# The ninth block of each probability tile: stored, and transposed together with those of other tiles

## The reference

```python
q_pool = q.reshape(B, H, S // 2, 2, D).mean(axis=3)
scores = scale * np.matmul(q_pool, k.transpose(0, 1, 3, 2))
scores = scores - np.max(scores, axis=-1, keepdims=True)
attn = np.exp(scores)
attn = attn / (np.sum(attn, axis=-1, keepdims=True) + 1e-09)
return np.matmul(attn, v)
```

## Time and profile before

| | us |
|---|---|
| Median of three runs | 989.16 |
| The profiled execution: device time | 988.49 |
| The profiled execution: span, first to last instruction | 986.7 |
| One pair, step 10 to step 10 (305.07 to 341.91) | 36.84 |
| TensorE busy in the span | 891.1 (90%) |
| VectorE busy | 597.8 (61%) |
| ScalarE busy | 497.0 (50%) |
| GpSimd busy | 294.5 (30%) |

### The profile page before, as it was taken

How to read it: one execution, slowest core, us unless ns; L and a number is a source line. 1 busy time by engine, 2 the same in 40 slices (tenths; PEclk the granted TensorE clock), 3 DMA queues, 4 the chain that set the end, 5 groups by cost and what they waited for, 6 DMA issues and landing times. The chain is left out here.

```text
span 986.7 us, 16399 instructions
## 1 busy us (share of the span) xinstructions
PE 891.1 (90%) x5707; PEld 644.4 (65%) x5707; DVE 597.8 (61%) x1175; ACT 497.0 (50%) x711; POOL 294.5 (30%) x207
## 2 busy tenths in 40 slices
PE   3999999999999999999999998876672899999998
PEld 2776776776776776776776765633231788888887
DVE  4676677677677677677677664420017866676770
ACT  1655555555555555555555553210016766666660
POOL 4353333333433333433433200000001343333441
PEclk9999999999999999999999999979885899999999
DMA  3312202202202202202202000949933100000000
GB/s 120 131 31 74 72 2 72 72 0 72 72 0 72 72 0 72 72 0 72 72 0 72 25 1 2 350 171 395 400 134 128 54 22 21 21 21 21 21 21 33
DMA packets 48865, 75.50 MB, mean 77 GB/s; under 512 B 5056, under 2 KB 23488, under 8 KB 48320
## 3 DMA queue, kind: packets, MB, share of 16 engines
q1 hardware_dynamic: 48832, 75.06, 22.3%
HBM read 70.32 MB, written 4.72 MB: 76 GB/s over the span
## 5 line engine op out<-in xcount | busy, mean ns | idle before, releaser
L496 DVE TENSOR_REDUCE part_neg<-ps 128x1 f32<-128x512 f32 (+1 forms) x432 | 220.8, 548 | 6.9 <-PE ps L304 6.6
L320 PE MATMUL ps<-ident,prob 128*128 128x128 f32 x1296 | 204.7, 285 | 19.1 <-DVE probT L415 9.2
L320 PEld LDWEIGHTS ps<-ident,prob 128*128 128x128 f32 x1296 | 143.2, 140 | 105.9 <-DVE probT L415 38.6
L415 DVE COPY probT<-ps 128x512 f32<-128x512 f32 (+1 forms) x256 | 125.1, 489 | 143.2 <-PE ps L320 116.8
L542 ACT ACTIVATE prob<-ps,neg_max 128x1152 f32<-128x1152 f32 x144 | 175.5, 1219 | 58.7 <-DVE neg_max L500 58.3
L304 PE MATMUL ps<-kT,qT_hi 128*128 128x512 f32 (+1 forms) x480 | 175.9, 383 | 5.3 <-DVE qT_lo L205 5.2
L553 ACT ACTIVATE probT<-ps 128x512 f32<-128x512 f32 x144 | 86.0, 597 | 171.6 <-PE ps L320 169.8
L337 PE MATMUL ps<-probT,v_nat 128*64 128x256 f32 (+1 forms) x1152 | 167.5, 417 | 0.5 <-DVE probT L415 0.5
L304 PE MATMUL ps<-kT,qT_lo 128*128 128x512 f32 (+1 forms) x480 | 159.3, 355 | 0.0
L1089 POOL TENSOR_TENSOR g_lo<-g,g_hi 128x1024 fp32r<-128x1024 f32 x36 | 86.5, 2404 | 134.7 <-ACT g_hi L1059 134.7
L1032 PE MATMUL ps<-w_hi,g_hi 128*128 128x512 f32 x288 | 113.9, 396 | 3.0 <-POOL g_lo L1089 3.0
(11 more groups left out here) (142 smaller groups left out, 1000.0 us busy)
## 6 DMA issues: line engine op xcount, KB each, us to landing
ring<-in_moe_w SPq DMA_DIRECT2D x10, 2048.0 KB, 20.1
k_nat<-in_k SPq DMA_DIRECT2D x16, 576.0 KB, 4.0
v_nat<-in_v SPq DMA_DIRECT2D x16, 576.0 KB, 5.2
q_nat<-in_q SPq DMA_DIRECT2D x32, 256.0 KB, 4.5
w_first<-in_moe_w SPq DMA_DIRECT2D x4, 2048.0 KB, 13.8
out<-res SPq DMA_DIRECT2D x18, 256.0 KB, 2.0
x<-in_moe_w SPq DMA_DIRECT2D x2, 2048.0 KB, 11.3
x<-in_moe_w_in SPq DMA_DIRECT2D x1, 4096.0 KB, 29.5
```

What stands on the lines that cost most here:

```text
L320: last = nc.tensor.transpose(block_at(s, kt), src[:, kt * P:(kt + 1) * P], ident[:])
L415: return eng_copy(probT[g][:, k0:k1, h, col:col + P], src.rearrange("p (c q) -> p c q", c=n))
L496: nc.vector.reduce_max(part_neg[:, c:c + 1], slot_banks(s)[:, c, 0:(CHUNK[c][1] - CHUNK[c][0]) * P], AX.X, negate=True).then_inc(part_done, 1)
```

## The change

The ninth block is no longer transposed with its tile. ACT copies it from `prob` to a new SBUF store, `stash` (one slot of 128x128 for each of the nine tiles), at the end of the step in which the tile's other blocks are transposed. The stored blocks are transposed in five groups ("tails"), all in steps that have no tile to transpose: in step 5 tiles 7 and 8 of the pair before and then tiles 0 and 1, in step 8 tiles 2, 3 and 4, in step 11 tiles 5 and 6. They go into `TBANK`, behind the new scores and ahead of the products with V, and wait for `out_evac` of that same step. ACT copies each group to `probT` with one instruction. DVE's third copy is gone. Where the step has new scores or K, the third chunk of these now waits for `second_evac`; in step 3 the second chunk of Q does.

```diff
+    TAILS = [(0, 1), (2, 3), (4,), (5, 6), (7, 8)]
+    TAIL_STEPS = {5: (0,), 8: (1, 2), 11: (3,), 17: (4,)}
+        stash = sb("stash", [P, TILES, P])
...
             def prob_chunk(p, par, j, s, c, out_before, tails_before):
                 tau = p * TILES + j
                 if c == 0:
                     wait(pe, exp_done, tau + 1)
                     wait(pe, first_evac, tau)
-                    if out_before is not None:
-                        wait(pe, out_evac, out_before)
-                elif c == 2:
-                    wait(pe, second_evac, tau + 1)
+                    wait(pe, tail_evac, tails_before)
+                    wait(pe, out_evac, out_before)
...
+            def tail_blocks(p, g, at):
+                for n, j in enumerate(TAILS[g]):
+                    wait(pe, stash_done, p * TILES + j + 1)
+                    last = nc.tensor.transpose(ps[:, TBANK, (at + n) * P:(at + n + 1) * P], stash[:, j, :], ident[:])
+                last.then_inc(tail_full, 1)
+                return at + len(TAILS[g])
...
             def pv(p, par, g, lo, hi):
-                    wait(pe, third_evac, tiles)
                 for m in range(lo, hi):
                     kt, h = PV_ORDER[m]
+                    if kt == TK and h == 0:
+                        wait(pe, tail_evac, p * NT + TAIL_OF[(G0 if g == 0 else TILES) - 1] + 1)
...
                         fill(0)
-                        fill(1)
-                    if tile2:
-                        prob_chunk(p - back, par ^ back, j, s, 2, None)
-                    if job:
-                        fill(2)
+                        for c in (1, 2):
+                            if tile2 and c == (1 if job[0] == "Q" else 2):
+                                wait(pe, second_evac, (p - back) * TILES + j + 1)
+                            fill(c)
+                    at = 0
+                    for b, tails in tails_at(s, first, last):
+                        if at == 0:
+                            wait(pe, first_evac, tiles_before(p, s, first, last))
+                            wait(pe, out_evac, outs_before(p, s + 1))
+                        for g in tails:
+                            at = tail_blocks(p - b, g, at)
                     for g, b, (lo, hi) in groups_at(s, PV_STEPS, first, last):
                         pv(p - b, par ^ b, g, lo, hi)
...
-                    def third():
-                        if t2 and t2[0] == "T":
-                            dve.wait_ge(ptr_full, (pp * TILES + j2) * NCH + 3)
...
-                            evac_chunk(nc.vector.tensor_copy, s, j2, 2).then_inc(third_evac, 1)
...
+            def tail_evacuate(n, at):
+                tiles = TAILS[n]
+                g, col = group_of(tiles[0]), column_of(tiles[0])
+                w = QR if tiles[0] == TILE.index(MIX) else P
+                nc.scalar.activation(probT[g][:, TK, :, col:col + w],
+                                     ps[:, TBANK, at * P:(at + len(tiles)) * P].rearrange("p (h q) -> p h q", h=2),
+                                     ACT.Copy).then_inc(tail_evac, 1)
...
                         consume(kind, n, p - back, par ^ back, s - 1)
+                    if t2 and t2[0] == "T":
+                        wait(act, tail_full, (pp - 1) * NT + TAIL_OF[j] + 1)
+                        nc.scalar.activation(stash[:, j, :], prob[prob_index(par ^ back2, j)][:, TK * P:S], ACT.Copy).then_inc(stash_done, 1)
+                    at = 0
+                    visit = [(p - b, n) for b, tails in tails_at(s, first, last) for n in tails]
+                    if visit:
+                        act.wait_ge(tail_full, visit[-1][0] * NT + visit[-1][1] + 1)
+                    for pq, n in visit:
+                        tail_evacuate(n, at)
+                        at += len(TAILS[n])
```

More of the change, by code:

```diff
@@ L55, in attention @@
     PV_LAST = [12, 19]
+    TAILS = [(0, 1), (2, 3), (4,), (5, 6), (7, 8)]
+    TAIL_STEPS = {5: (0,), 8: (1, 2), 11: (3,), 17: (4,)}
+    TAIL_OF = {j: n for n, tiles in enumerate(TAILS) for j in tiles}
+    NT = len(TAILS)
+    TK = CHUNK[2][0]
     OUT_STEP = [17, 23]
@@ L152, in groups_at, with tails_at, tail_count, tiles_before @@
                     yield g, 1, table[g][s + STEPS]
+        def tails_at(s, first, last):
+            if s < STEPS and s + STEPS in TAIL_STEPS and not first:
+                yield 1, TAIL_STEPS[s + STEPS]
+            if s in TAIL_STEPS:
+                yield 0, TAIL_STEPS[s]
+        def tail_count(p, s):
+            later = sum(len(v) for k, v in TAIL_STEPS.items() if k >= s + STEPS)
+            return (p - 1) * NT + NT - later + sum(len(v) for k, v in TAIL_STEPS.items() if k < s)
+        def tiles_before(p, s, first, last):
+            done = [job_at(k, 2, first, last) for k in range(s)]
+            kind, j, back = [t for t in done if t and t[0] == "T"][-1]
+            return (p - back) * TILES + j + 1
+        def outs_before(p, s):
+            return (p - 2) * 2 + sum(1 for b in range(3) for so in OUT_STEP if so - STEPS * b < s)
         def steps_of(last):
@@ L340, in pv, with out_chunk @@
                     last.then_inc(pv_done, 1)
-            def out_chunk(p, g, tiles_before):
+            def out_chunk(p, g, tiles_before, tails):
                 pe.wait_ge(pv_evac, p * 2 + g + 1)
                 wait(pe, first_evac, tiles_before)
+                wait(pe, tail_evac, tails)
                 wait(pe, out_evac, p * 2 + g)
@@ L375, in body @@
                         _, j, back = tile2
[L376 to L381, removed]
+                        out_before = outs_before(p, s)
                         for c in (0, 1):
-                            prob_chunk(p - back, par ^ back, j, s, c, out_before)
+                            prob_chunk(p - back, par ^ back, j, s, c, out_before, tail_count(p, s))
                     for g in range(2):
@@ L386, in body @@
                             if OUT_STEP[g] == s + STEPS * b and not (b and first):
-                                done = [k for k in range(s + 1) if job_at(k, 2, first, last) and job_at(k, 2, first, last)[0] == "T"]
-                                jj = job_at(done[-1], 2, first, last)
-                                out_chunk(p - b, g, (p - jj[2]) * TILES + jj[1] + 1)
+                                out_chunk(p - b, g, tiles_before(p, s, first, last), tail_count(p, s))
                     if job:
@@ L535, in consume @@
                     act.wait_ge(neg_done, tau + 1)
-                    wait(act, ptr_full, (tau - 1) * NCH)
+                    wait(act, ptr_full, (tau - 1) * 2)
+                    wait(act, stash_done, tau - 1)
                     if n == 0:
@@ L556, in body @@
                         kind, n, back = prev
-                        t3 = job_at(s, 3, first, last)
-                        if kind != "T" and t3 and t3[0] == "T":
-                            wait(act, third_evac, (p - t3[2]) * TILES + t3[1] + 1)
                         consume(kind, n, p - back, par ^ back, s - 1)
+                    if t2 and t2[0] == "T":
[8 more added lines that the diff above has]
+                        at += len(TAILS[n])
                     for g in range(2):
```

38 lines of the change are left out of this document (12 added, 26 removed).

## The result

The changed kernel takes **1011.11 us** (median of four runs, 1008.33 to 1017.12) where the kernel before, beside it, takes 988.96: the ratio is 1.0217, 95% interval 1.0183 to 1.0251. It is slower by 22 us. The forecast was 1004 us, slower, in a range of 992 to 1012: the result lies 0.9 us inside the high end.

What follows compares the result with a forecast made beforehand. TensorE, 97.58 of 100 us busy, was taken to bound the attention; 0.96 + 0.45 + 0.17 - 0.53 = +1.05 us a pair, +15.8 for fifteen pairs, ends -1, so +15: 1004 us, range 992 to 1012.

Steps and rivals of the forecast that it cites:

- the signs that were named: Waits in steps 11 and 3, steps 1 and 6 at 2.55, steps 5 and 8 longer, a pair of 37.9 us.
- those that would have made it wrong: Steps 1 and 6 shorter than 2.55, no wait in step 11, or step 0 falling by 0.16 or more.
- The blocks: Nine tail blocks transposed in steps 5, 8 and 11, all on the path: +0.96 us a pair.
- Step 11's wait: Tails in step 11 wait for VectorE to read the output out of TBANK: +0.45 us a pair, bounds 0.2 and 0.6.
- Step 5's wait: In step 5 VectorE's output read ends in time, 0.2 earlier after the change: no cost.
- The Q step: In step 3 Q's second chunk waits for second_evac: +0.17 us a pair, bounds 0 and 0.25.
- The ninth block removed: Taking it from its tile in steps 0, 2, 4, 7 and 9 saves 0.53 us a pair; second_evac's wait stays.
- ScalarE: Its copies to the store and out of TBANK, about 4.4 us more a pair, are covered and cost nothing.
- VectorE's relief: Nine copies of 285 ns go; nobody on the path waits for them outside step 2 and 0.19 in step 11.
- The ends: Last pair and drain: waits give back about 2 us, last tails and output read take about 1: net -1.

Runs made afterwards that it cites:

- e10: Changed kernel with group 1's output read ahead of tile 7's last maximum, reciprocal in step 3, Q's wait before its last block: 997.88 us, ratio 1.0078.
- e7: Changed kernel without the tails' transposes, copies and waits, so the last 128 keys are left out of the products with V: 985.4 us, ratio 0.9937.
- e5: Changed kernel with VectorE's read of group 1's output ahead of tile 7's last maximum and neg_max: 1005.25 us, ratio 1.0153.
- e9: Changed kernel without tails, copies to the store, or VectorE's copy of the second four blocks and TensorE's wait for it: 973.46 us.
- e2: Changed kernel with row_den and its reciprocal computed in step 3 instead of step 5: 1010.3 us, ratio 1.019.
- e3: Changed kernel with step 3's wait for VectorE's copy before the last block of Q's second chunk, not its first: 1008.4 us, ratio 1.0195.
- e8: Changed kernel without the tails and without ScalarE's copies to the store: 981.89 us, ratio 0.9904.
- e6: Changed kernel with an unawaited 128x128 VectorE copy put back where its third copy was, in six steps: 1016.02 us, ratio 1.0246.
- e12: Kernel before, with the products with V ahead of the ninth block and last chunk in steps 0, 2, 4, 7 and 9: 982.01 us, ratio 0.9924.
- e11: Kernel before, with the products with V ahead of the ninth block and K's last chunk in step 9: 985.12 us, ratio 0.995.
- e1: Changed kernel with the tails of steps 5 and 11 behind the first four products with V: 1010.05 us, ratio 1.0198.

## Why the prediction was right, and where it fell short

The sign and the mechanism held; the size was short by a quarter to a third: +1.05 us a pair was forecast, +1.42 came. That the range held was in part luck, since the result lies 0.9 us inside its end. Of the signs that were named, the waits in steps 11 and 3 and the 2.55 us of steps 1 and 6 came; none of those that would have made it wrong did. Term by term:

- **The blocks**: 0.96 forecast, 1.06 measured (e10 against e7). Each block costs 0.118, not the 0.106 of a row of eight; that the rest is what the start and end of such a group cost is likely, but no run shows it.
- **Step 11's wait**: 0.45 forecast, 0.48 measured (e5). This was read from the rows of before, with its cause, and held. Beside it there are up to 0.06 us between the output transposes and the scores (0.22 after, 0.16 before), in e7 too: the wait for ScalarE's copy of K, told under e9.
- **Step 5's wait**: "In step 5 the same wait ends in time" is the step that failed; e2 measures 0.15 us a pair (2.3 us in all), and the mean of 13 pairs hides that they alternate. Two errors are in it. I compared the read's end with the products' start at 328.58, but behind scores the products stand off by a gap that transposes don't have: the tails are ready about 0.1 earlier (2.63 us into the step in e2, where the products began at 2.72 before). And I let VectorE's relief carry the read 0.2 forward, when in this step VectorE is held by GpSimd, whose work did not move forward: the read ends 2.62 or 2.76 us into the step, by turns, and 2.56 before.
- **The Q step**: 0.17 forecast, 0.18 measured (e3). Step 3 lay at 2.73, where the Trainium skill's rule on a change of the tiling mode (TensorEngine Tiling (Array Packing), section Key Properties) would have put it at 2.80. After the wait the four Q blocks take 0.59 to the small ones and these 0.27 to the next tile, together 0.86, where six blocks in a row would take about 0.7 (6 x 0.118, from eight Q blocks in 0.95 us): this case shows about 0.15 for both ends together, and doesn't split them.
- **The ninth block removed**: 0.53 forecast; the steps of e8 against the means of before give 0.51 (0.07, 0.07 and 0.06 in steps 0, 4 and 7, 0.14 in step 2, 0.17 in step 9). Step 10 is 0.07 shorter too, but step 11 gives 0.06 of it back; I counted nothing for step 10, for another reason (that the wait in step 11 swallows it). That the kept wait would eat half of the saving was said; e9 shows it.
- **ScalarE**: nothing forecast, nothing found (e8 for the copies to the store; the five out of `TBANK` have no run of their own). It is busy 3.1 us more a pair, where 4.4 were forecast. **VectorE's relief**: worth only what the text gave it (e6).
- **The ends**: -1 forecast, +0.8 measured. From the last pair's step 5 to the gating stage are 34.16 us before, 32.18 in e7 and 34.96 after. So the waits for the ninth block gave back 2.0, as forecast, and the last tails and their output read, which I put at 1, cost 2.8. The rows from the drain, where the tails wait for the read of the output that was just transposed:

```profile
634.25 0.27 PE L382 MATMUL ps<-ident,outT 128*64 128x128 f32 x1
...
634.97 0.27 DVE L492 TENSOR_TENSOR x<-ps,row_inv 64x128 f32<-64x128 f32 x1
...
635.35 0.41 PE L350 MATMUL ps<-ident,stash 128*128 128x128 f32 x2 [0.82 <-issue]
```

Together the terms of a pair as measured are 1.06 + 0.48 + 0.15 + 0.18 - 0.51 = 1.36 of the 1.42.

The steps held by the exp kept their length: steps 1 and 6 stayed at 2.55 in every run (step 1 in e12 apart), and TensorE's waits for the exp behind them grew, from 0.17 to 0.23 and from 0.28 to 0.39 us, by what it had saved. The blocks moved out of them (three of nine, counting step 3) had to be paid in full elsewhere, and so had step 10's. That is the core of the loss even with all waits repaired: e10 is still 0.58 us a pair above before, of which four blocks at 0.118 are 0.47; the other five cost 0.59 and gave back 0.51.

## What to carry to other kernels

Before work is moved off an engine's crowded places, ask what it costs where it is: in a step held by another engine it is free, and anywhere else it is not. For each buffer that the moved work shares, find who frees it and what that engine does first; then compare with the moment at which the moved instruction is ready, not with the instruction that stood there before it. In this kernel one wait was taken away by changing the order on the engine that ends it (e5), and one by moving covering work in front of it (e11), for less than by moving the waiting work.

## What the runs showed of the hardware

**A small VectorE instruction can wait out a GpSimd instruction.** `row_den` (128x10) takes 0.16 us in step 3 (e2). Beside GpSimd's `qT_hi` it took 1.23: from 337.85 to 339.08, and `qT_hi` ran from 336.83 to 339.04. The kernel before shows it too:

```profile
325.09 2.21 POOL L203 TENSOR_TENSOR qT_hi<-q_raw,ones 128x1216 fp32r<-128x1216 f32 x1 [12.61 <-PE ps L304]
...
326.30 1.03 DVE L447 TENSOR_SCALAR row_den<-row_sum 128x10 f32<-128x10 f32 x1
```

It ended at 327.33, `qT_hi` at 327.30. In the last pair of that kernel, where no `qT_hi` runs, it takes 0.16 (at 584.07). The trace counts the time as busy, not as a wait. The Trainium skill (SBUF — State Buffer, section Who interferes with whom) says that VectorE and GpSimd share a pair of SBUF ports which one instruction holds to its end, and that tensor_scalar is among the VectorE instructions that can take it; the trace agrees for this one. The reciprocal behind it, at 0.22 us, isn't held up in either kernel; but it starts about 0.01 us before GpSimd's next instruction, so this row doesn't tell whether it could be.

**Going between products (64 output rows a tile) and transposes has a price.** In e1 it was 0.25 us for there and back (step 11 3.78, against 3.53 in e5); in e11, with the products between K's blocks and the ninth block, the step is 0.37 shorter, more than the wait of 0.22 that it covers. The price depends on what stands on both sides, and these runs don't give a rule.

**A wait in front of a weight load costs more than the matmul row shows.** With the copy done at about the time it is needed (324.11, the load at 324.16), TensorE shows no idle time at the matmul, yet each such place costs 0.12 us (e9, where the load starts 0.23 us ahead of its pass). That the copy is done early doesn't always win this back: in e12 it was done 1.36 us ahead and the step gained 0.02.
